# Attention and a mixture of experts on one core: near scores ahead of the last transpose, softmax in halves, first weights loaded in the loop, rows stored at the end

## The chip, the cores and the metric

One core of one Trainium2 chip runs the whole kernel. The time is that of the device, in microseconds (us), from start to end of the program. Short names: PE is TensorE, PEld its weight loads, DVE VectorE, ACT ScalarE, POOL GpSimd, SP SyncE, whose queue issues most transfers.

## The reference, cut to what matters

Two stages, in float32. The attention has 4 batches, 8 heads, 576 positions and heads of 64; it adds a pooled attention (q, k and v averaged over 4 positions, 144 x 144 scores) and a near one (each position sees those less than 4 away). The mixture routes each of 2304 rows to one of 8 experts.

```python
q_d, k_d, v_d = (mean of 4 positions of q, k, v)
out_up = np.repeat(sm_attn(q_d, k_d, v_d), 4, axis=2)
scores = np.where(abs(i - j) < 4, scale * q @ k.T, -1e9)
x = out_up + softmax(scores) @ v            # (4, 576, 512)
logits = x @ w_gate                          # 8 experts, and a local gate
e = argmax(logits) or the previous row's e, by the local gate
out = p[e] * (relu(x @ w1[e]) @ w2[e])       # w1 512 x 1024, w2 1024 x 512
```

## The kernel before, in words

The attention is cut into 16 units, each a batch and a pair of heads. `body(u)` stands once on each engine: unit 0 is written out, units 1 to 14 run in a loop of two bodies, unit 15 is written out. The engines run side by side and meet only at semaphores; on each engine the order is that of the code.

On PE a body is: pool scores of u (L1153); transposes 0 and 1 of unit u+1 (q of the two heads, L1143); near values of u-1 (L1232); transpose 2 (k); the near mask laid into PSUM (L1169); transpose 3; near scores of u on top of the mask (L1179); pool transposes (L1193); `repeat` of u-1 (L1244), which spreads the pooled output over 4 positions; pool values (L1217); near transposes (L1203). Transpose g writes the PSUM bank of its head, so transpose 2 waits for the copies of transpose 0 and transpose 3 for those of transpose 1.

ACT copies the transposes out (L656 for q, four copies a unit; L658 for k, two), takes the exponentials (`exp_pool` L664, `exp_near` L671) and copies their transposes (`pool_out` L678, `near_out` L684). DVE takes maximum and difference of the pool scores (L822, L825) and of the near ones (L833, L836), scales outputs (L857, L846) and adds both outputs into `xs` (`x_out`, L867). POOL adds four neighbours for pooled q and k (`pool_qk`, L489 and L491, once for q and once for k) and v (`pool_v`, L501, L505), and splits the pooled output (`split_opool`).

Every product whose left rows are `float32` and must be exact is made of two parts, hi and lo. The weights of expert 0 are loaded into `w_ring` (`load_w1(0)` L367, `load_w2(0)` L373), and their split runs in 8 pieces of 1024 columns: `first_hi` on ACT (L726), then `first_lo` on POOL (L591). Their place is that of the attention's buffers, so piece 0 waits until q and k of all units are transposed. Between attention and experts stand the logits: 32 steps, each a transpose (`x_chunk`, L1307), a copy on ACT (L732), a difference on DVE (L921) and a product (L1317); every fourth a product back (L1325). Then a chain of small DVE operations finds each row's slot, POOL gathers rows from `x_rows` (L601), and PE runs the experts (L1405). `x_rows` is written by 48 stores of SP (L409).

`keep_warm` (L1126) is a number of products that nobody reads; WARM, WARM_FIRST and WARM_TILES say how many.

Of the kernel before, what the change touches and what calls it, by code (L numbers as in the profile page):

```python
# [34 lines left out]
def build(nc, q, k, v, w_gate, w_local, w1, w2, out):  # L35
# [3 lines left out]
    POOL = 4  # L39
# [56 lines left out]
    WARM, WARM_FIRST, WARM_TILES = 12, 6, 16  # L96
# [3 lines left out]
    with ctx:  # L100
# [159 lines left out]
        s_qk_in = [sem("s_qk_in0"), sem("s_qk_in1")]  # L260
# [62 lines left out]
        def _(sp):  # L323
            def load_qk(u, par):

                wait(sp, s_tr, 4 * (u - 1))
                for h in range(2):
# [3 lines left out]
                                 ).then_inc(s_qk_in[par], 16)  # L331
                for h in range(2):
                    sp.dma_start(k_in[:, par, :, h, :],
                                 ku[one(u), h, :, :].rearrange("o (t p) d -> p (o t) d", p=QT)
                                 ).then_inc(s_qk_in[par], 16)
# [51 lines left out]
            with sp.Fori(2, UNITS // 2) as kk:  # L387
# [6 lines left out]

            sp.dma_start(gates_w[:, :, 0:E], w_gate.rearrange("(c p) e -> p c e", p=128)).then_inc(s_wg, 16)
# [37 lines left out]
        def _(pool):  # L433
# [45 lines left out]
            def pool_qk(u, par):  # L479

                for a in range(2):

                    wait(pool, s_tr_out, COPIES * u + copied[2 * a + 1])
                    if isinstance(u, int) and u == 0:
                        pool.wait_ge(s_tr_odd, a + 2)
# [35 lines left out]
            pool_qk(0, 0)  # L521
# [62 lines left out]
            split_opool(UNITS - 1)  # L584
            constants()

            for i in range(FPIECES):
# [3 lines left out]
                nc.gpsimd.tensor_tensor(lo, lo.bitcast(F32), hi.bitcast(F32), ALU.subtract).then_inc(s_first_lo, 1)  # L591

# [53 lines left out]
        def _(act):  # L646
# [20 lines left out]
            def exp_near(u):  # L667

                wait(act, s_cenn, u + 1)
                wait(act, s_ptn, 2 * u)  # L670
                nc.scalar.activation(p_near[:, :, :, 0:WIN].rearrange("p t h w -> p h t w"), cen_near[:],  # L671
                                     ACT.Exp, scale=SCALE).then_inc(s_expn, 1)

            def pool_out(u):
                wait(act, s_opool, u)
                for h in range(2):
                    wait(act, s_ptp, 2 * u + h + 1)
                    nc.scalar.copy(pt_pool[:, h, :], bank[TBANK[h]][0:PC + 1, 0:GW]).then_inc(s_ptp_out, 1)  # L678
# [7 lines left out]

            def body(u, par, t=True):
# [28 lines left out]
            def first_hi(i):  # L716

                at = i * FCOL
                act.wait_ge(s_w1_in if at < W1C else s_w2_in, 16)
                if i == 0:  # L720
# [772 lines left out]
```

## Time and profile before

| | us |
|---|---|
| runs: median (lowest to highest) of 3 | 500.35 (500.07 to 501.8) |
| the profiled execution: its own time, its span | 502.7, 501.0 |
| start to the end of body 0 | 19.5 |
| bodies 1 to 14 (the loop) | 107.1 |
| body 15 until the last `x_out` | 18.3 |
| logits | 24.4 |
| routing until the first expert product | 29.8 |
| experts | 301.8 |

The stages are cut where PE or DVE begins the next one's first instruction. PE is busy 92% of the span, DVE 51%, ACT 43%, POOL 38%. A time in a row is counted from the start of the span; "L" is a line of the kernel before.

### The profile page before, as it was taken

The numbers are of one execution on the slowest core, as the hardware profiler recorded it, in microseconds if no ns is written. First come the engines' busy times: TensorE is split into PE (matmuls) and PEld (weight loads), VectorE is DVE, ScalarE is ACT, GpSimd is POOL, SyncE is SP. The second block draws the span as 40 slices with busy tenths as digits, with TensorE's granted clock in tenths as the row PEclk, the third lists the DMA queues.
The fourth block names the chain that finished last, engine by engine and source line by source line (L and its number), as shares of the span: only waits on it lengthen the run. The fifth ranks groups of instructions, "written<-read, shape, count | busy, mean of one in ns | idle before, by whom it ended". The sixth has DMA issues, their size and how long they took to land.

```text
span 501.0 us, 13091 instructions
## 1 busy us (share of the span) xinstructions
PE 462.3 (92%) x4156; PEld 371.0 (74%) x4163; DVE 257.0 (51%) x383; ACT 217.3 (43%) x377; POOL 192.7 (38%) x252
## 2 busy tenths in 40 slices
PE   7999999999889558999999999999999999999981
PEld 3787787788667325788888888888888888888860
DVE  3577777677556686353453452345346473522220
ACT  2666767767347220254244252525427282512220
POOL 7777677676459202113204213221321514042200
PEclk9999999999889867999999999999999999999997
DMA  8866665664966732215326421642646564121100
GB/s 179 171 151 161 174 159 149 172 155 92 353 175 149 253 122 43 22 44 211 139 90 230 146 82 48 211 153 78 211 156 231 170 245 156 69 73 35 36 26 6
DMA packets 85936, 69.22 MB, mean 138 GB/s; under 512 B 47886, under 2 KB 70926, under 8 KB 85904
## 3 DMA queue, kind: packets, MB, share of 16 engines
q1 hardware_dynamic: 81408, 57.78, 39.3%
q0 software_dynamic: 4496, 11.03, 7.1%
q8 instruction: 18, 0.29, 0.2%
q14 instruction: 14, 0.11, 0.1%
HBM read 59.34 MB, written 10.76 MB: 140 GB/s over the span
## 4 chain that ended last, share of the span: by engine, by line
PE 77%; DVE 9%; ACT 7%; issue 5%; POOL 1%; ACTq 0%; POOLq 0%; DVEq 0%
PE psum L1405 51%; PE psum L1423 4%; ACT early L656 4%; PE psum L1143 3%; PE psum L1126 3%; PE psum L1203 2%; DVE early L836 2%; DVE top_near L833 2%; PE psum L1179 2%; ACT early L671 2%; PE psum L1153 2%; PE psum L1383 2%; PE psum L1307 2%; PE psum L1317 1%; PE psum L1325 1%
## 5 line engine op out<-in xcount | busy, mean ns | idle before, releaser
L1405 PE MATMUL psum<-w_ring,xg_t 128*128 x552 | 133.9, 398 | 2.3 <-DVE xg_t L1065 1.6
L1405 PE MATMUL psum<-w_ring,h_t 128*128 x552 | 134.3, 398 | 1.9 <-issue 1.9
L1405 PEld LDWEIGHTS psum<-w_ring,xg_t 128*128 128x128 f32 x552 | 102.2, 188 | 25.0 <-issue 2.7
L1405 PEld LDWEIGHTS psum<-w_ring,h_t 128*128 128x128 f32 x552 | 102.0, 188 | 25.0 <-issue 2.4
L607 POOL DMA_INDIRECT out<-tile_bufs,to_row x23 | 23.5, 1024 | 197.3 <-DVE tile_bufs L1080 197.3
L1053 DVE TENSOR_TENSOR w_ring<-w_ring (+1 forms) x28 | 62.9, 2287 | 25.8 <-ACT w_ring L746 25.8
L767 ACT ACTIVATE tile_bufs<-psum 128x512 f32<-128x512 f32 x46 | 25.0, 596 | 86.9 <-PE psum L1405 86.8
L1065 DVE TENSOR_TENSOR xg_t<-psum,xg_t 128x512 fp32r<-128x512 f32 x24 | 16.5, 690 | 84.1 <-ACT xg_t L760 84.1
L746 ACT CAST w_ring<-w_ring (+1 forms) x28 | 52.1, 1910 | 17.4 <-DMA w_ring<-moe_w 17.4
L774 ACT CAST h_t<-psum 128x512 fp32r<-128x512 f32 x46 | 24.8, 591 | 76.3 <-PE psum L1423 76.2
L1080 DVE TENSOR_SCALAR tile_bufs<-psum,slot_w 128x512 f32<-128x512 f32 x23 | 17.2, 749 | 58.2 <-PE psum L1405 58.2
L601 POOL DMA_INDIRECT tile_bufs<-x_rows,from_row x24 | 26.0, 1083 | 36.3 <-DVEq L1020 27.1
L615 POOL DMA_INDIRECT slot_w<-w_rows,from_row x23 | 26.2, 1137 | 17.5 <-DMA w_rows<-weight 10.7
L489 POOL TENSOR_TENSOR early<-early 128x288 f32<-128x288 f32 x32 | 21.3, 665 | 26.3 <-ACT early L656 22.8
L656 ACT COPY early<-psum 64x288 f32<-64x288 f32 x60 | 25.0, 417 | 13.9 <-PE psum L1143 12.8
L1071 DVE TENSOR_TENSOR h_t<-psum,h_t 128x512 fp32r<-128x512 f32 x46 | 29.5, 683 | 2.1 <-ACT h_t L774 1.8
L1143 PE MATMUL psum<-ident,early 96*128 96x96 f32 x192 | 27.1, 263 | 1.9 <-ACT early L707 0.2
L1143 PEld LDWEIGHTS psum<-ident,early 96*128 96x128 f32 x192 | 18.4, 143 | 12.0 <-ACT early L656 6.0
L1423 PE MATMUL psum<-ident,tile_bufs 128*128 128x128 f32 x184 | 23.9, 273 | 0.3 <-ACT tile_bufs L767 0.3
L1423 PEld LDWEIGHTS psum<-ident,tile_bufs 128*128 128x128 f32 x184 | 21.4, 141 | 3.7 <-ACT tile_bufs L767 0.5
L1126 PE MATMUL psum<-warm 128*128 128x512 bf16 x60 | 21.5, 516 | 2.4 <-POOL warm L441 1.4
L760 ACT CAST xg_t<-psum 128x512 fp32r<-128x512 f32 x24 | 14.2, 593 | 19.2 <-PE psum L1383 19.2
(179 smaller groups left out, 613.4 us busy)
## 6 DMA issues: line engine op xcount, KB each, us to landing
w_ring<-moe_w SPq DMA_DIRECT2D x16, 2048.0 KB, 9.1
early<-q SPq DMA_DIRECT2D x32, 144.0 KB, 2.5
early<-k SPq DMA_DIRECT2D x32, 144.0 KB, 3.1
early<-v SPq DMA_DIRECT2D x16, 288.0 KB
x_rows<-early SPq DMA_DIRECT2D x48, 96.0 KB, 2.5
early<-v SPq DMA_DIRECT2D x32, 120.0 KB
early<-v SPq DMA_DIRECT2D x64, 13.5 KB
early<-v SPq DMA_DIRECT2D x32, 15.0 KB
```

The source lines that it names most:

```text
L601: pool.indirect_dma_start(xg[:, t % 2, :], None, x_rows[:, :], bass.IndirectOffsetOnAxis(from_row[:, t:t + 1], 0), bounds_check=NTOK - 1, ...
L615: pool.indirect_dma_start(slot_w[:, t:t + 1], None, w_rows[:, :], bass.IndirectOffsetOnAxis(from_row[:, t:t + 1], 0), bounds_check=NTOK - ...
L656: nc.scalar.copy(q_of(par, g, e), q_transposed(g, e)).then_inc(s_tr_out, 1)
L746: nc.scalar.copy(w_ring[:, bass.ds(at + i * n, n)], w_ring[:, bass.ds(at + (WCOLS + i * n), n)].bitcast(F32)).then_inc(s_hi, 1)
L767: nc.scalar.activation(h_act[:, n * 512:(n + 1) * 512], bank[1 + n][:, :], ACT.Relu).then_inc(s_relu, 1)
L774: nc.scalar.copy(h_t[:, 0, n * 512:(n + 1) * 512], bank[3 + n][:, :]).then_inc(s_ht_hi, 1)
L1053: nc.vector.tensor_tensor(part, part.bitcast(F32), w_ring[:, bass.ds(at + i * n, n)].bitcast(F32), ALU.subtract).then_inc(s_lo, 1)
L1071: nc.vector.tensor_tensor(h_t[:, 1, n * 512:(n + 1) * 512], bank[3 + n][:, :], h_t[:, 0, n * 512:(n + 1) * 512].bitcast(F32), ALU.subtract ...
L1126: mm(bank[b][:, :], warm[:, 0:128], warm[:, :], start=True, stop=True)
L1143: last = nc.tensor.transpose(bank[TBANK[h]][:, j * QT:(j + 1) * QT], rows, ident[0:QT, 0:QT])
L1405: ins = mm(bank[b][:, :], rows, w_ring[:, bass.ds(at + (off + c * width + n * 512), 512)], start=(c == 0 and k == 0), stop=(c == chunks - ...
L1423: last = nc.tensor.transpose(bank[3 + n][:, c * 128:(c + 1) * 128], h_act[:, (4 * n + c) * 128:(4 * n + c + 1) * 128], ident[:])
```

## The change

- Near scores follow the mask at once; transpose 3 comes behind them.
- Maximum, difference and exponential of the near scores run in two halves of three tiles; on ACT `pool_out` and `exp_near` alternate by halves, on PE the near transposes and the pool values wait by halves, and `repeat` is cut around the pool transposes.
- q and k have semaphores of their own, so the first q transposes don't wait for k.
- DVE makes the pooled q and k of unit 0, in place of POOL.
- Eight in place of twelve opening warm-up products, four in place of six in each of two places of body 0 (the second cut into two and two).
- `load_w1(0)` and `load_w2(0)` are issued between turns of the load loop, behind the loads of units 7 and 11. `first_hi` 0 to 2 run in body 15, 3 to 5 early in the logits, 6 and 7 behind the logits' exponential; `first_lo` 0 and 1 run ahead of the last `split_opool`.
- All 48 stores wait for the last `x_out`; before, those of a batch waited for that batch.

```diff
-    WARM, WARM_FIRST, WARM_TILES = 12, 6, 16
+    WARM, WARM_FIRST, WARM_TILES = 8, 4, 16
...
+            with sp.Fori(2, 4) as kk:
+                two_units(kk)
+            load_w1(0)
+            with sp.Fori(4, 6) as kk:
+                two_units(kk)
+            load_w2(0)
+            with sp.Fori(6, UNITS // 2) as kk:
+                two_units(kk)
...
-            load_w1(0)
-            load_w2(0)
...
+            sp.wait_ge(s_x, UNITS)
             for b in range(NB):
-                wait(sp, s_x, HP * (b + 1))
...
-            pool_qk(0, 0)
             pool_v(0, 0, 0)
...
+            first_lo(0)
+            first_lo(1)
+            split_opool(UNITS - 1)
+            constants()
+            for i in range(2, FPIECES):
+                first_lo(i)
...
+            def exp_near(u, j):
+                tiles = slice(j * HALF, (j + 1) * HALF)
+                wait(act, s_cenn, 2 * u + j + 1)
                 wait(act, s_ptn, 2 * u)
...
+                else:
+                    first_hi(0)
                 exp_pool(u)
+                if not t:
+                    first_hi(1)
...
-                pool_out(u)
-                exp_near(u)
+                for j in range(2):
+                    pool_out(u, j)
+                    exp_near(u, j)
+                if not t:
+                    first_hi(2)
                 near_out(u)
...
+                if k == 1:
+                    first_hi(3)
+                    first_hi(4)
+                elif k == 8:
+                    first_hi(5)
             act.wait_ge(s_cent, 1)
...
+            first_hi(6)
+            first_hi(7)
...
+                for j in range(2):
+                    tiles = slice(j * HALF, (j + 1) * HALF)
+                    nc.vector.reduce_max(top_near[:, :, tiles], s4[:, :, tiles], X).then_inc(s_topn, 1)
+                    wait(dve, s_topn, 2 * u + j + 1)
+                    nc.vector.tensor_tensor(cen_near[:, :, tiles], s4[:, :, tiles],
...
+            for a in range(2):
+                dve.wait_ge(s_tr_out, copied[2 * a + 1])
+                dve.wait_ge(s_tr_odd, a + 2)
+                t4 = qk_t[:, 0, a, :].rearrange("p (s r) -> p s r", r=POOL)
+                nc.vector.tensor_tensor(qk_part[:, a, :, :], t4[:, :, 0:2], t4[:, :, 2:4], ALU.add).then_inc(s_part, 1)
...
                 near_masked(u, par)
+                near_scores(u, par)
                 if t:
                     transposes(3, u + 1, 1 - par, nxt)
-                near_scores(u, par)
-                pool_transposes(u, t)
-                if x:
-                    repeat(u - 1)
-                else:
-                    keep_warm(WARM_FIRST, 7)
+                for j in range(2):
+                    if x:
+                        repeat(u - 1, j, HALF if j else 1)
+                    else:
+                        keep_warm(WARM_FIRST // 2, 7)
+                    pool_transposes(u, j, t)
                 pool_values(u, par)
                 near_transposes(u)
```

PE's order in a body of the loop, before, from the mask (L1169) to the pool transposes and `repeat` (L1244); `L32` rows are waits' registers:

```order
L1169 MATMUL psum<-mask,ident_b 112x324 x2
L32 REGISTER_ALU
L1143 MATMUL psum<-ident,early 128x96 x3
L1179 MATMUL psum<-early 48x54 x24
L32 REGISTER_ALU
L1193 MATMUL psum<-ident,early 72x72 x2
L1193 MATMUL psum<-ident,early 73x72 x2
L32 REGISTER_ALU
L1193 MATMUL psum<-ident,early 72x72 x2
L1193 MATMUL psum<-ident,early 73x72 x2
L1244 MATMUL psum<-o_pool_r,rep_r 112x256 x6
```

The same place now; mask L1209, near scores L1219, transpose L1183, `repeat` L1284, pool transposes L1232:

```order
L1209 MATMUL psum<-mask,ident_b 112x324 x2
L1219 MATMUL psum<-early 48x54 x24
L32 REGISTER_ALU
L1183 MATMUL psum<-ident,early 128x96 x3
L1284 MATMUL psum<-o_pool_r,rep_r 112x256 x2
L32 REGISTER_ALU
L1232 MATMUL psum<-ident,early 72x72 x2
L1232 MATMUL psum<-ident,early 73x72 x2
L1284 MATMUL psum<-o_pool_r,rep_r 112x256 x4
L32 REGISTER_ALU
L1232 MATMUL psum<-ident,early 72x72 x2
L1232 MATMUL psum<-ident,early 73x72 x2
```

The 24 near scores moved ahead of a transpose of 3, and one third and two thirds of `repeat` stand before the first and the second half of the pool transposes.

ACT's order now in body 15 and the first logit steps; L712 is `first_hi`, L691 `pool_out`, L685 `exp_near`, L697 `near_out`, L754 the logits' copy:

```order
L712 CAST w_ring<-w_ring 128x1024
L691 COPY pt_pool<-psum 73x288
L685 ACTIVATE early<-early 112x2x3x54
L691 COPY pt_pool<-psum 73x288
L685 ACTIVATE early<-early 112x2x3x54
L712 CAST w_ring<-w_ring 128x1024
L697 COPY pt_near<-psum 128x336 x2
L754 CAST x_t<-psum 128x288 x2
L712 CAST w_ring<-w_ring 128x1024 x2
L754 CAST x_t<-psum 128x288 x7
L712 CAST w_ring<-w_ring 128x1024
L754 CAST x_t<-psum 128x288 x23
```

Before, the pieces (L726) stood one by one between the logits' copies (L732), up to the last of them:

```order
L726 CAST w_ring<-w_ring 128x1024
L732 CAST x_t<-psum 128x288 x3
L726 CAST w_ring<-w_ring 128x1024
L732 CAST x_t<-psum 128x288 x5
L737 ACTIVATE expo<-e_buf 112x192
```

Three pieces moved up into body 15, three stand early in the logits, two fall behind L737.

## Rows read from the trace of the kernel before

**Rows 1.** Busy time by stage: length, engines (PE first), granted clock, DMA share, GB/s.

```profile
0.00:19.52 19.52, 15.66 (x139) 9.34 (x142) 7.60 (x19) 7.98 (x18) 13.88 (x36) 1.00 0.87 181
19.52:126.61 107.09, 102.62 (x2158) 85.64 (x2160) 79.48 (x126) 73.36 (x167) 77.79 (x115) 1.00 0.63 152
126.61:144.91 18.30, 15.78 (x234) 12.34 (x237) 10.06 (x18) 6.23 (x15) 6.37 (x25) 0.81 0.92 310
144.91:169.35 24.44, 22.04 (x178) 17.59 (x177) 14.44 (x36) 16.69 (x34) 18.95 (x8) 1.00 0.57 139
```

**Rows 2.** Chain that ended last, one body of the loop: start, us, what.

```profile
91.85 0.76 PE psum L1179 x48
...
92.64 0.84 DVE top_near L833
...
94.37 0.76 ACT early L671
```

**Rows 3.** Timeline of PE, the same body.

```profile
90.82 0.44 PE L1169 MATMUL psum<-mask,ident_b 112*112 112x324 bf16 x2
91.38 0.47 PE L1143 MATMUL psum<-ident,early 96*128 96x96 f32 x3
...
93.85 1.19 PE L1217 MATMUL psum<-v_pool,pt_pool 72*72 72x65 f32 x16
95.25 0.79 PE L1203 MATMUL psum<-ident,early 112*128 112x112 f32 x6 [0.20 <-ACT early L671]
95.97 0.47 PE L1153 MATMUL psum<-early 64*72 64x144 f32 x4
```

**Rows 4.** Timeline of ACT and DVE, the same body.

```profile
91.35 0.69 ACT L664 ACTIVATE early<-early 72x576 f32<-72x576 f32 x1
...
90.88 0.96 DVE L857 TENSOR_TENSOR o_near<-psum,r_near 112x768 f32<-112x768 f32 x1
```

**Rows 5.** Timeline, start of the kernel.

```profile
1.40 5.30 PE L1126 MATMUL psum<-warm 128*128 128x512 bf16 x12 [1.40 <-POOL warm L441]
...
8.79 0.46 DVE L899 COPY early<-psum 128x288 f32<-128x288 f32 x1 [0.62 <-PE psum L1143]
...
10.88 0.71 PE L1153 MATMUL psum<-early 64*72 64x144 f32 x8 [1.26 <-POOL early L491]
...
19.52 0.71 PE L1153 MATMUL psum<-early 64*72 64x144 f32 x8 [0.84 <-POOLq L535]
```

**Rows 6.** Chain that ended last, body 15 and the logits.

```profile
132.68 1.28 issue
133.96 1.11 PE psum L1217 x8
...
139.25 1.47 PE psum L1232 x48
...
155.28 0.28 ACT w_ring L726
```

**Rows 7.** Transfers that SP issued, in order of time.

```profile
110.00 0.83 SPq L329 DMA_DIRECT2D early<-q  x2
...
125.15 3.49 SPq L409 DMA_DIRECT2D x_rows<-early  x1
...
154.98 9.74 SPq L409 DMA_DIRECT2D x_rows<-early  x15
166.75 0.37 SPq L367 DMA_DIRECT2D w_ring<-moe_w  x1
```

**Rows 8.** Timeline, logits to the first gather.

```profile
144.55 1.05 ACT L726 CAST w_ring<-w_ring 128x1024 fp32r<-128x1024 f32 x1
...
174.69 1.90 ACT L746 CAST w_ring<-w_ring 128x2048 fp32r<-128x2048 f32 x1 [3.78 <-DMA w_ring<-moe_w]
...
193.29 1.26 POOL L601 DMA_INDIRECT tile_bufs<-x_rows,from_row  x1 [27.09 <-DVEq L1020]
...
197.62 0.58 ACT L760 CAST xg_t<-psum 128x512 fp32r<-128x512 f32 x1 [19.23 <-PE psum L1383]
```

More of the change, by code:

```diff
@@ L386, in _, with two_units @@
             load_v_raw(3, 1)
-            with sp.Fori(2, UNITS // 2) as kk:
+            def two_units(kk):
                 load_v_win(2 * kk - 2, 0)
@@ L583, in _, with first_lo @@
             pool.sem_inc(s_gates, 1)
-            split_opool(UNITS - 1)
-            constants()
-            for i in range(FPIECES):
+            def first_lo(i):
                 pool.wait_ge(s_first_hi, i + 1)
@@ L685, in near_out, with first_hi @@
                                    bank[TBANK[j]][:, 0:TW]).then_inc(s_ptn_out, 1)
+            def first_hi(i):
+                at = i * FCOL
+                act.wait_ge(s_w1_in if at < W1C else s_w2_in, 16)
+                if i == 0:
+                    act.wait_ge(s_tr, 4 * UNITS)
+                elif i == 3:
+                    act.wait_ge(s_vpool, UNITS)
+                    act.wait_ge(s_pooled, 2 * UNITS)
+                elif i == 6:
+                    act.wait_ge(s_onear, UNITS)
+                nc.scalar.copy(w_ring[:, at:at + FCOL],
+                               w_ring[:, WCOLS + at:WCOLS + at + FCOL].bitcast(F32)).then_inc(s_first_hi, 1)
             def body(u, par, t=True):
@@ L733, in _ @@
                                rows_of(bank[XBANK[k]])).then_inc(s_xt_hi, 1)
-                if k % 3 == 2 and 4 <= k and k // 3 - 1 < FPIECES:
-                    first_hi(k // 3 - 1)
+                if k == 1:
[3 more added lines that the diff above has]
+                    first_hi(5)
             act.wait_ge(s_cent, 1)
@@ L1128, in transposes @@
             def transposes(g, u, par, half):
-                wait(pe, s_qk_in[par], 64 * (half + 1))
                 if g < 2:
+                    wait(pe, s_q_in[par], 32 * (half + 1))
                     wait(pe, s_ptn_out, 2 * (u - 2) + g + 1)
                 else:
+                    wait(pe, s_k_in[par], 32 * (half + 1))
                     wait(pe, s_tr_out, COPIES * u + copied[g - 2])
@@ L1146, in pool_scores @@
             def pool_scores(u, par):
-                wait(pe, s_cenn, u)
+                wait(pe, s_cenn, 2 * u)
                 wait(pe, s_pooled, 2 * u + 2)
@@ L1208, in pool_values @@
             def pool_values(u, par):
-                wait(pe, s_ptp_out, 2 * u + 2)
                 wait(pe, s_vpool, u + 1)
                 wait(pe, s_onear_out, u)
-                for qc in range(2):
-                    for h in range(2):
+                for h in range(2):
+                    wait(pe, s_ptp_out, 2 * u + 1 + h)
+                    for qc in range(2):
                         c0 = (qc * 2 + h) * VW
@@ L1235, in near_values, with repeat @@
                 last.then_inc(s_onear, 1)
-            def repeat(u):
-                wait(pe, s_osplit, 2 * u + 2)
-                wait(pe, s_x, u)
-                for i in range(HALF):
+            def repeat(u, first=0, end=HALF):
+                if first == 0:
+                    wait(pe, s_osplit, 2 * u + 2)
+                    wait(pe, s_x, u)
+                for i in range(first, end):
                     for part in range(2):
@@ L1245, in repeat @@
                                   o_pool_r[:, part, :], start=(part == 0), stop=(part == 1))
-                last.then_inc(s_rep, 1)
+                if end == HALF:
+                    last.then_inc(s_rep, 1)
             def body(u, par, half, t=True, x=True):
@@ L1340, in _ @@
             pe.wait_ge(s_gates, 1)
-            pe.wait_ge(s_cenn, UNITS)
+            pe.wait_ge(s_cenn, 2 * UNITS)
             logit_step(0, 1)
```

70 lines of the change are left out of this document (27 added, 43 removed).

## The prediction

> **What bounds the kernel now.** I cut the profile by stages first, since the edits sit in four of them [rows 1]. The start takes 19.52 us, the loop 107.09 for 14 bodies (7.65 each), body 15 until the last sum into xs 18.30, the logits 24.44. The reader is to see PE busy 102.62 of 107.09 in the loop. So a body has little idle PE time to give back, and PE's own work is the floor of whatever is gained there.
>
> Second, the chain of waits inside a body. It leaves PE at the end of the near scores (91.85 + 0.76 = 92.61), runs over DVE twice (maximum and difference, 0.84 each), over ACT (0.76), and comes back to PE for the near transposes [rows 2]. PE does other things meanwhile, so third its timeline [rows 3]: where does it really stand still? At two places. The mask starts at 90.82 and the transpose behind it, which waits for ACT's copies of the q transposes, only at 91.38. And the pool values, 1.19 from 93.85, end at 95.04, but the near transposes start at 95.25, released by ACT.
>
> Fourth, body 15, which takes 18.30 where a body of the loop takes 7.65. The reader is to see a hole of 1.28 put down to "issue", in the middle of 16 like products with no wait between them, and behind it products at half speed: the near values take 1.47 [rows 6], and the granted clock of the stage is 0.81 on average [rows 1]. In this stage DMA is at 0.92 of its time and moves 310 GB/s, against 152 in the loop: the two first weight loads, 4 MB, are under way.
>
> **The start.** Twelve warm-up products take 5.30 from 1.40, 0.44 each [rows 5]; eight end 1.7 earlier, near 4.9, and the first transposes no longer wait for k. Their duration at the low clock doubles for the first six, which eats a part, so I put DVE's last copy of k (ends 9.25 [rows 5]) at 7.8. The pooled sums come behind it on DVE. Its price is read from the 288-element copy (0.46 [rows 5]) and the 648-element maximum (0.84 [rows 2]): 1.06 ns an element and 0.15 fixed. Two sums of 288 and two of 144 elements are then 1.5 to 1.6, and pool scores 0 start near 9.5 in place of 10.88: 1.4 gained. Body 1 does not begin by PE's own work: it waits for POOL (L535, at 19.52 [rows 5]), which makes its constants behind the k sums of unit 1, and these now hang on a transpose that comes behind the near scores, some 0.25 later in the body. **1.1 us gained**; bounds 2.0 gained (POOL freed earlier) and 1.0 lost (the clock comes later).
>
> **The loop.** With near scores straight behind the mask, DVE can begin when they end: mask at 90.82 plus about 0.34, near scores 0.76, so 91.92. DVE is busy with `o_near` until 90.88 + 0.96 = 91.84 [rows 4], just in time. Halves of 324 elements cost 0.50 each by the slope above, so the four end at 92.4, 92.9, 93.5 and 94.0; that is 0.33 more DVE work, in a body where it is busy 79.48 / 14 = 5.7 of 7.65. ACT: 576 elements take 0.69 [rows 4] and 648 0.76 [rows 2], so half of them about 0.48. With the `pool_out` halves between, the two exponentials end near 93.8 and 94.65. PE meanwhile: transpose 3 (0.47 less an overlap of 0.07), pool transposes, `repeat` and pool values, which before took from 92.61 to 95.04, 2.43. They end at 91.92 + 0.40 + 2.43 = 94.75. The first near transposes need the first exponential (93.8), the second, begun near 95.1, the second (94.65). So neither of the two stops is left, with 0.4 to spare at the tighter one.
>
> What PE gains is its idle time and no more. First stop: 0.56 from start to start in place of 0.34, 0.2. Second: 1.40 from start to start in place of 1.19 less the 0.07 by which modelled ends overlap the next start (95.25 + 0.79 against 95.97 [rows 3]), 0.28. I take 0.45 of the 0.5, since waits are now taken by halves: 7.20 a body, **6.3 us gained** over 14. Bounds: only the first stop goes (0.2, so 2.8) and 0.6 a body (8.4). Transpose 3 itself comes later by near scores, but its copy on ACT stands behind the pool exponential, which ends at 91.35 + 0.69 = 92.04 [rows 4], and one k copy, so 92.4 as before: no cost while that cover stands, at most 0.4 of POOL's slack if not.
>
> **Body 15.** The weights are now loaded behind units 7 and 11, eight and four bodies ahead of where their neighbours in the queue stood, so DMA is nearly idle here. I take the 1.28 hole for something that full DMA queues cause, instructions that come late among them, and the low clock for its consequence; the trace shows them only together. Laid out with the durations of the loop, PE ends the near transposes 7.3 after the body's start. `first_hi` 0 and 1 (1.05 each [rows 8]) fall in ACT's idle time before and behind the pool exponential. `first_hi` 2 does not: it holds `near_out` until 8.5. Then one logit transpose (0.45), four warm-ups (0.9, at half their opening 0.44 each) and near values (0.83, a little over half of the 1.47) end at 10.7. From there to the last `x_out` it took 144.91 - 140.72 = 4.2 before, and nothing there changes. 14.9 against 18.3: **3.4 us gained**. Bounds: 0.5 and 4.5. `first_lo` 0 and 1 hold the last `split_opool` by some 2 us, hidden by near values, as `repeat` 15 comes two logit steps later.
>
> **The logits.** ACT carries 8 pieces of 1.05 among 32 copies, and twice the chain runs over such a piece [rows 6, 8]. The first costs about its 1.05; at the second a group of four steps takes some 0.7 longer. Now two pieces stand before near values end, one at the ninth copy, and two behind the exponential where ACT waits anyway. **1.7 us gained**; bounds 1.0 and 2.5.
>
> **The late stores.** The last `x_out` would end at 144.9 - 1.1 - 6.3 - 3.4 = 134.1. An undisturbed store costs 9.74 / 15 = 0.65 of SP [rows 7]; 48 end at 165.3. Before, w1 of expert 1 was issued 2.0 behind the last store, and ACT began to split it at 174.69, 7.9 later [rows 7, 8]. So ACT splits from 175.2 to 179.0. It is needed for the first gathered rows at 197.62 - 12.5 = 185.1, and the gather itself at 180.8 needs stores landed by then; they have been since 167. Nothing lost, with 6 us to spare; without that cover each 0.1 a store costs 4.8.
>
> **Sum.** 1.1 + 6.3 + 3.4 + 1.7 = 12.5. The profiled execution took 502.7, its span 501.0, so it becomes 490.2. It stands 2.35 above the median of the runs, 500.35; the forecast for the median is 487.9.
>
> **Rivals.**
> - *The hole in body 15 stays.* For it: the cut is inside straight-line code just behind a loop, which the change keeps. Against: the like code of the logits has no such hole, at 139 GB/s. Then 1.28 and the half-speed products behind it return, together the 3.4, and the gain is 9.1: 491.3. The Trainium skill (Runtime: NRT & Kernel Launch, Instruction fetch mechanics) says that the fetch of the next block of straight-line code is mostly hidden, which would speak for another cause and so for this rival; the row shows the hole and not what it waited for.
> - *Halves cost what they give.* More instructions and waits on DVE and ACT keep one PE stop: 0.2 a body, gain 9.0: 491.4. Against: DVE has over a microsecond idle in a body.
> - *The weights push the units' loads.* Each is 2.1 MB, 6.8 us at the 310 GB/s of the stage that had them [rows 1]. q of unit 15 was issued at 110.00 [rows 7] and is used in body 14, which starts at 126.61 - 7.65 = 118.96, 0.64 in. Less 0.8 to issue and 2.5 to land (the page's median for q) 6.3 are spare, 5.4 at the new pace. SP itself was held 3.49 by the two loads [rows 7]. If both add up, 3.5 + 6.8 - 5.4 = 4.9 a load: 497.7. The Trainium skill (DMA: Bandwidth & Descriptors, Queues, rings and completion order) says that an engine takes descriptors in ring order; by it whatever follows a weight waits for all of it. Against the full sum: q is issued some 5 us behind the weight, so most of it has passed.
> - *The clock comes late.* Eight warm-ups may not carry it through body 0; it then runs at 1.2 GHz and costs some 5: 493. The rows show only that twelve did.
> - *The late stores decide,* the one on the other side. Stores, landing, load and split of expert 1's w1 then stand ahead of ACT's first gathered rows. It turns the sign at (197.6 - 3.8 - 7.9 - 2.0 - 134.1) / 48 = 1.04 a store. For it: the first store took 3.49 [rows 7]. Against: that was behind 4 MB, and fifteen free ones took 0.65 each. At 1.15 a store, 505 for the profiled execution: 503.
>
> **Chances.** Forecast 0.66, the hole 0.12, halves 0.08, pushed loads 0.07, late clock 0.04, late stores 0.03. The first three rivals and the unknown costs of the loop (-2.1 to +3.5) set the range: 483.5 to 495.5. What a measurement of this kernel tells from no change is about 0.5%, 2.5 us. Pushed loads at nearly their full price end within it, and so does a late clock with a second rival; the late stores end above. Faster 0.91, same 0.06, slower 0.03.
>
> **What would show it.** Body to body 7.2 in the loop; no PE stop before the near transposes; four DVE rows of about 0.50 with 324 elements; transposes starting near 4.9 and pool scores near 9.5; no hole in body 15 and a granted clock near 1.0 there; DMA full for 5 to 6 us twice in the loop with PE unmoved; stores from about 134 to 165 and 9 us or more between their landing and the first gather. The prediction is wrong if PE waits for loads in the loop, if PE's order costs more than the sum of its products, or if the expert stage starts by ACT's split and not by the gather.

## The result, and the profile after

The changed kernel takes 507.39 us (median of 20 runs, 501.23 to 517.76) against 500.28 for the kernel before (20 runs, 499.13 to 503.05). Its range is four times as wide. The ratio is 1.0085, interval 1.0059 to 1.0110; it leaves out the executions that lie over 1.5% above the fastest of their kernel (7 of the 20 here; the median of the other 13 is 504.37), which is why it is smaller than that of the medians. So the change makes the kernel slower, by 0.9%. Where two versions are compared below, the ratios decide, and a difference of medians stands beside them only to tell the size.

The profiled execution took 504.37, its span 502.6, against 502.7 and 501.0 before. It lies 3 us below the median of all 20, so the trace shows a mild case. The mean granted clock of all 20 executions goes with their time: 0.960 in the one of 501.23, 0.922 in the one of 517.76.

The same stages as in [rows 1], kernel after (length; busy time of PE, PEld, DVE, ACT, POOL; granted clock; DMA share; GB/s):

```profile
0.00:18.45 18.45, 13.13 (x132) 8.04 (x134) 9.18 (x25) 8.11 (x19) 11.71 (x32) 1.00 0.89 177
18.45:128.66 110.21, 105.11 (x2158) 88.86 (x2158) 82.84 (x154) 76.78 (x181) 77.26 (x114) 0.94 0.85 186
128.66:143.46 14.80, 13.11 (x235) 10.39 (x237) 10.41 (x21) 10.63 (x21) 12.80 (x29) 1.00 0.01 2
143.46:166.47 23.01, 21.84 (x178) 17.58 (x177) 14.49 (x35) 11.18 (x27) 8.22 (x4) 1.00 0.54 133
```

| stage | before | after | difference |
|---|---|---|---|
| start, until body 1 | 19.52 | 18.45 | -1.07 |
| bodies 1 to 14 | 107.09 | 110.21 | +3.12 |
| body 15 until the last sum into xs | 18.30 | 14.80 | -3.50 |
| logits | 24.44 | 23.01 | -1.43 |
| routing, until the first product of expert 0 | 29.82 | 34.36 | +4.54 |
| experts | 301.83 | 301.77 | -0.06 |
| span | 501.0 | 502.6 | +1.6 |

Three stages went as forecast. Two did not: the loop, which should have given 6.3, and the routing, which the prediction did not touch. The reader is to see the loop's granted clock, 0.94 where it was 1.00.

**An undisturbed body.** From body to body the 14 took 9.98, 7.40, 7.17, 7.12, 7.19, 7.13, 8.66, 7.10, 7.18, 7.11, 12.74, 7.11, 7.19 and 7.10. Ten lie between 7.10 and 7.19. PE in one of these, the same place as [rows 3] (start, us, engine, line, operation, output<-inputs, shape, count):

```profile
45.47 0.44 PE L1209 MATMUL psum<-mask,ident_b 112*112 112x324 bf16 x2
45.84 0.79 PE L1219 MATMUL psum<-early 64*48 64x54 f32 x48
...
48.23 1.38 PE L1256 MATMUL psum<-v_pool,pt_pool 72*72 72x65 f32 x16
49.45 0.74 PE L1242 MATMUL psum<-ident,early 112*128 112x112 f32 x6
```

and DVE's four halves in the same body:

```profile
46.99 0.50 DVE L863 TENSOR_REDUCE top_near<-psum 112x6 f32<-112x324 f32 x1 [0.51 <-PE psum L1219]
47.52 0.50 DVE L865 TENSOR_TENSOR early<-psum,top_near 112x324 f32<-112x324 f32 x1
47.94 0.48 DVE L863 TENSOR_REDUCE top_near<-psum 112x6 f32<-112x324 f32 x1
48.45 0.49 DVE L865 TENSOR_TENSOR early<-psum,top_near 112x324 f32<-112x324 f32 x1
```

No bracket of a wait stands on the PE rows: both stops of before are gone, and a half costs the 0.50 that was forecast.

**The three long bodies.** PE's timeline of after; the bracket gives the idle time ahead of the row and what ended it:

```profile
18.45 1.24 PE L1193 MATMUL psum<-early 64*72 64x144 f32 x8 [2.27 <-POOLq L543]
...
20.77 1.55 PE L1271 MATMUL psum<-early,pt_near 55*48 55x65 f32 x48
...
66.32 0.86 PE L1183 MATMUL psum<-ident,early 96*128 96x96 f32 x6 [1.16 <-DMA early<-q]
67.11 0.90 PE L1271 MATMUL psum<-early,pt_near 55*48 55x65 f32 x48
...
98.65 1.22 PE L1183 MATMUL psum<-ident,early 96*128 96x96 f32 x6 [3.45 <-DMA early<-q]
99.80 1.55 PE L1271 MATMUL psum<-early,pt_near 55*48 55x65 f32 x48
```

Two of the three wait for q. The near values (L1271) take 0.90 in a free body. Behind the first and the third stop they take 1.55, as in other stretches at a granted clock of 0.50, and behind the second 0.90. So the stop of 1.16 costs its body only 8.66 - 7.15 = 1.5, with a wait of 0.24 for k behind it, and the stop of 3.45 costs 12.74 - 7.15 = 5.6: the wait, and the products at 1.2 GHz behind it. Why q is late stands in SP's timeline of after, behind the first weight load (L367):

```profile
52.53 0.41 SPq L367 DMA_DIRECT2D w_ring<-moe_w  x1
...
54.26 0.94 SPq L356 DMA_DIRECT2D early<-v  x2
55.38 2.22 SPq L350 DMA_DIRECT2D early<-v  x2
57.79 1.07 SPq L356 DMA_DIRECT2D early<-v  x2
59.14 2.74 SPq L329 DMA_DIRECT2D early<-q  x2
```

and in the windows of after around both loads (columns as above):

```profile
50.00:55.00 5.00, 5.00 (x130) 4.02 (x128) 3.89 (x7) 4.06 (x10) 3.35 (x6) 1.00 1.03 201
55.00:60.00 5.00, 5.00 (x96) 4.23 (x94) 4.26 (x10) 3.66 (x10) 4.09 (x6) 1.00 1.01 354
60.00:65.00 5.00, 5.00 (x97) 4.31 (x95) 4.05 (x8) 4.06 (x10) 4.11 (x7) 1.00 1.23 220
65.00:70.00 5.00, 3.60 (x115) 2.78 (x112) 2.77 (x5) 2.81 (x7) 2.37 (x5) 1.00 0.94 160
...
97.00:103.00 6.00, 4.35 (x83) 3.52 (x87) 1.19 (x2) 2.73 (x6) 1.09 (x2) 0.50 0.91 175
```

The weight itself costs SP only 0.41. But from about 55 to 61 the DMA engines move 284 to 397 GB/s where they moved 183 in the body before (44.3 to 51.5), and issuing a pair of q loads takes 2.74 where it took 0.83 [rows 7]. This q is that of unit 8: it is issued 6.6 behind the weight and ends the stop at 66.32, 4.4 behind the end of its issue, where the median of all q loads is 2.9. The DMA share by itself tells less. It stands at 0.94 or more from 50 to 70, but it was 0.90 in the body before the load, and in e7 (below) the same unit loads show 0.92 for 25 us, from 41 to 66, with no pair of issues over 1 us and no stop of PE. The last row has the granted clock around the second stop for q, 0.50.

**The routing.** POOL and DVE of after, just behind the logits:

```profile
169.05 4.64 POOL L597 TENSOR_TENSOR w_ring<-w_ring 128x1024 fp32r<-128x1024 f32 x2 [17.36 <-ACT w_ring L712]
169.06 2.37 DVE L992 TENSOR_TENSOR keep<-keep,later 112x24 f32<-112x24 f32 x1
171.46 2.25 DVE L993 TENSOR_SCALAR keep<-keep,valid 112x24 f32<-112x24 f32 x1
173.75 0.18 DVE L994 TENSOR_TENSOR fresh<-fresh,keep 112x24 f32<-112x24 f32 x1
```

The same two operations, in the kernel before:

```profile
171.94 0.18 DVE L953 TENSOR_TENSOR keep<-keep,later 112x24 f32<-112x24 f32 x1
172.16 0.24 DVE L954 TENSOR_SCALAR keep<-keep,valid 112x24 f32<-112x24 f32 x1
```

POOL's two operations are the residuals (`first_lo`) of pieces 6 and 7, which the change puts behind the logits' exponential. Each DVE operation begins beside one of them (2.34 the first, and 4.64 both) and lasts until it ends: 4.62 for what took 0.42. These 4.2 are nearly the whole of the stage's +4.54.

**The late stores.** SP, ACT and POOL of after:

```profile
143.48 33.25 SPq L420 DMA_DIRECT2D x_rows<-early  x48
178.82 0.40 SPq L367 DMA_DIRECT2D w_ring<-moe_w  x1
...
186.71 3.70 ACT L772 CAST w_ring<-w_ring 128x2048 fp32r<-128x2048 f32 x2 [16.80 <-DMA w_ring<-moe_w]
...
194.84 1.26 POOL L614 DMA_INDIRECT tile_bufs<-x_rows,from_row  x1 [21.15 <-DVEq L1059]
```

48 stores take 33.25 / 48 = 0.69 each. ACT's split ends at 190.4, and the first gather starts at 194.84 behind DVE, so neither stores nor split decide in this trace.

### The profile page after: what moved, and what is told of

The parts are those of the page before. It is cut to its first block, busy times and chain, and to the rows that moved or that the text cites. A ratio compares the mean times of both kernels' runs of the same rounds, so it can differ in the third digit from the quotient of the medians.

```text
span 502.6 us, 13207 instructions
## 1 busy us (share of the span) xinstructions
PE 459.0 (91%) x4148; PEld 371.1 (74%) x4155; DVE 267.3 (53%) x419; ACT 221.5 (44%) x393; POOL 189.8 (38%) x248
## 4 chain that ended last, share of the span: by engine, by line
PE 73%; SPq 11%; DVE 6%; issue 4%; DMA 3%; POOL 1%; ACT 1%; POOLq 0%; DVEq 0%
PE psum L1447 51%; PE psum L1465 4%; SPq L356 3%; SPq L350 3%; PE psum L1425 2%; PE psum L1183 2%; SPq L329 2%; PE psum L1349 2%; SPq L333 2%; PE psum L1271 2%; PE psum L1359 1%; PE psum L1256 1%; DMA early<-v 1%; PE psum L1367 1%; PE psum L1219 1%
## 5 line engine op out<-in xcount | busy, mean ns | idle before, releaser
L1183 PE MATMUL psum<-ident,early 96*128 96x96 f32 x192 | 28.5, 273 | 5.3 <-DMA early<-q 4.6
L498 POOL TENSOR_TENSOR early<-early 128x288 f32<-128x288 f32 x30 | 20.0, 665 | 28.1 <-ACT early L669 20.3
L1183 PEld LDWEIGHTS psum<-ident,early 96*128 96x128 f32 x192 | 19.2, 149 | 12.7 <-issue 8.7
L597 POOL TENSOR_TENSOR w_ring<-w_ring 128x1024 fp32r<-128x1024 f32 x8 | 18.7, 2364 | 17.7 <-ACT w_ring L712 17.4
L1256 PE MATMUL psum<-v_pool,pt_pool 72*72 72x65 f32 (+1 forms) x256 | 22.1, 231 | 0.2 <-ACT pt_pool L691 0.2
```

The costliest lines, as they stand in the source:

```text
L1183: last = nc.tensor.transpose(bank[TBANK[h]][:, j * QT:(j + 1) * QT], rows, ident[0:QT, 0:QT])
L1256: last = mm(bank[4][0:PC, c0:c0 + VW], pt_pool[0:PC + c, h, at:at + PC], v_pool[0:PC + c, par, h, c, :], start=(c == 0), stop=(c == 1))
```

## The experiments

The theory had three parts: the two weight loads in the loop cost most, by late q loads and the clock that falls behind them (the late loads); the last two residuals hold DVE, 4.2 us (the held DVE); PE's stop before body 1 lets the clock fall, 2.8 us (the early stop). Against it stood that the new order of the loop costs the time itself, and, for the late loads, that only the order within SP's queue is at fault, or only the size of a transfer. The kernel before ran beside each of them, with medians of 500.19 (the first four runs), 500.21 (the next two), 500.57 (the next four) and 500.75 (the last two).

| run | median | range, runs | ratio to before, interval |
|---|---|---|---|
| e1_weights_back | 492.73 | 491.01 to 499.97, 6 | 0.9848, 0.9802 to 0.9894 |
| e2_split_early | 503.20 | 497.43 to 508.26, 12 | 1.0012, 0.9979 to 1.0046 |
| e3_reps_first | 504.41 | 500.93 to 511.40, 12 | 1.0057, 1.0028 to 1.0086 |
| e4_pieces | 500.20 | 499.01 to 505.58, 12 | 1.0015, 0.9986 to 1.0044 |
| e5_before_loads | 505.80 | 504.39 to 506.37, 6 | 1.0108, 1.0088 to 1.0127 |
| e6_all_three | 499.16 | 492.51 to 501.52, 6 | 0.9892, 0.9854 to 0.9931 |
| e7_repairs | 490.48 | 489.97 to 491.44, 5 | 0.9804, 0.9782 to 0.9827 |
| e8_stores_staged | 490.79 | 488.92 to 491.20, 5 | 0.9801, 0.9777 to 0.9826 |
| e9_act_queue | 509.71 | 502.84 to 513.72, 8 | 1.0066, 1.0035 to 1.0097 |
| e11_warm_back | 495.02 | 493.76 to 498.13, 6 | 0.9893, 0.9864 to 0.9923 |
| e12_loop_alone | 494.15 | 493.96 to 495.65, 6 | 0.9879, 0.9857 to 0.9902 |

**e1: the weight loads and their splits where they were before, the rest of the change kept.**

```diff
-            with sp.Fori(2, 4) as kk:
-                two_units(kk)
-            load_w1(0)
-            with sp.Fori(4, 6) as kk:
-                two_units(kk)
-            load_w2(0)
-            with sp.Fori(6, UNITS // 2) as kk:
+            with sp.Fori(2, UNITS // 2) as kk:
                 two_units(kk)
...
             load_v_win(UNITS - 1, 1)
+            load_w1(0)
+            load_w2(0)
...
+                if k % 3 == 2 and 4 <= k and k // 3 - 1 < FPIECES:
+                    first_hi(k // 3 - 1)
```

> The changed kernel with the first weight loads and all eight first splits back where the kernel before has them (loads behind the load loop, pieces among the logits); late stores and everything else of the change stay. Theory A (the weight loads in the loop hold up q and k of later units, and two of the late split pieces on POOL stretch two tiny DVE operations to 2.4 and 2.3 us): no PE wait for q in the loop, bodies 2 to 14 all 7.1 to 7.2 us, the two tiny DVE operations back at 0.2 us; body 15 again near 18 us with its hole; profiled execution near 497.5 us, and the times of its runs within 1% of each other. Rival B (the loop reordered by halves is itself what stalls, by PE waits that wander): single bodies of 8 to 13 us stay, and the time stays above 502. Rival C (nothing but SP's own pace holds the loop): bodies between 7.2 and 7.6 with SP never waiting.

Measured: 492.73, 14.7 below the changed kernel by the medians and 2.4%, some 12 us, by the ratios. No wait for q or k is left in the loop, and 12 of its 14 bodies take 7.11 to 7.19. The two DVE operations take 0.18 and 0.24 again. The run takes away the late loads and the held DVE together and does not price them apart. SP's timeline of e1 up to the q of the same unit 8:

```profile
59.40 0.76 SPq L350 DMA_DIRECT2D early<-v  x2
60.34 0.80 SPq L356 DMA_DIRECT2D early<-v  x2
61.41 0.83 SPq L329 DMA_DIRECT2D early<-q  x2
```

This q is issued 7.9 ahead of body 7, which uses it, and in after only 5.3 ahead. The new order of the loop is that of the changed kernel, and it pays. The early stop shows too: PE still stops 2.51 before body 1, and in the traced execution (499.97, above the median) the clock stays down for two bodies, 11.83 and 9.92. A body 15 near 18 did not come: it takes 14.97.

**e2: pieces 6 and 7 split at the 13th and 17th copy of the logits.**

```diff
-                elif k == 8:
-                    first_hi(5)
+                elif k in (8, 12, 16):
+                    first_hi({8: 5, 12: 6, 16: 7}[k])
...
-            first_hi(6)
-            first_hi(7)
```

> The changed kernel with first_hi 6 and 7 moved from behind the logits' exponential to the 13th and 17th logit copy, so that POOL has split the last piece before the routing begins. Theory A: the DVE operations of lines 992 and 993 (0.2 us each in the kernel before, 2.38 and 2.27 in the changed one) last as long because POOL works at two pieces then; they are back at 0.2, routing takes 29.8 us in place of 34.4, and the logits at most 0.7 more: 4 us off the changed kernel's profiled 504.4. Rival: they wait for something else that runs at that time (ACT's copies of the same pieces, or code that comes late): the two stay at 2.3 each and nothing is gained.

Measured: 503.20, 4.2 below the changed kernel by the medians and 3.7 by the ratios, whose intervals lie apart. The routing takes 29.69 in place of 34.36, the two operations 0.18 and 0.24, and the logits stay at 23.05, where after had 23.01. So the held DVE is shown, and the split could have gone early at no price. The loop has its q waits as before, of 1.49 and 3.17.

**e3: POOL makes the constants of `repeat` ahead of the first pooled v.**

```diff
-            pool_v(0, 0, 0)
-            pool_qk(1, 1)
-
             grid = rep[:].rearrange("p t (s r) -> p t s r", s=2)[:, :, :, 0:QS]
...
             pool.sem_inc(s_reps, 1)
+
+            pool_v(0, 0, 0)
+            pool_qk(1, 1)
```

> The changed kernel with POOL's repeat constants made while POOL waits for v of unit 0, ahead of its first pool_v. Theory A: PE stood still 2.27 us before body 1 because POOL made them behind the k sums of unit 1, and that idle time is what dropped the clock to 1.2 GHz for body 1 (10.05 us in place of 7.15): body 1 starts near 16.2 in place of 18.45 and takes 7.2 to 7.6 at full clock; 4.5 to 5 us off, unless the loads of the loop then take some of it back. Rival: the clock falls anyhow, for want of the warm-up products taken out (4 and 6 fewer): body 1 starts near 16.2 and still takes 10.

Measured: 504.41; the ratio, 1.0057, is not clearly apart from that of the changed kernel. Body 1 starts at 16.37 without a stop and takes 7.20, so the early stop has its cause in POOL's order. But the late loads take this back in the trace: body 7 starts 4.9 earlier than in after, the q that it needs is issued only 3.0 earlier, at 56.14. PE's timeline of e3:

```profile
64.15 1.22 PE L1183 MATMUL psum<-ident,early 96*128 96x96 f32 x6 [3.90 <-DMA early<-q]
...
67.31 0.74 PE L1209 MATMUL psum<-mask,ident_b 112*112 112x324 bf16 x2
```

The wait was 1.16 in after; here it is 3.90, the mask behind it takes 0.74 in place of 0.44, and the body 15.76.

**e4: each weight load in four pieces of 512 KB, one behind the loads of each of units 6 to 13.**

```diff
-            load_w1(0)
...
+                if i is not None:
+                    piece(i)
```

> The changed kernel with each first weight load cut into four of 512 KB, one issued behind the loads of each of units 6 to 13. Theory A (a 2 MB load in the queue holds back what is issued behind it, and PE then waits for q): no q wait over 0.5 us in the loop and no fall of the clock there, 7 us off, and runs closer together than 501 to 518. Rival (SP's queue has no room for 4 MB more in the loop however it is cut: 6.5 us of issuing a unit in a body of 7.2): SP falls behind piece by piece, and a wait of some us returns in bodies 10 to 14; less than 3 us off.

Measured: 500.20. More waits (0.53, 0.48, 1.38 and 1.56), none as long as 3.45, and bodies 10 to 13 take 8.19, 8.62, 11.99 and 9.55. Against the changed kernel this is 7.2 less by the medians but 3.5 by the ratios, about half of the 7 that were expected if size alone were at fault. So a smaller transfer helps, but the backlog is spread and not removed.

**e5: the kernel before, with only its two weight loads moved into the load loop.**

```diff
+            with sp.Fori(2, 4) as kk:
+                two_units(kk)
+            load_w1(0)
+            with sp.Fori(4, 6) as kk:
+                two_units(kk)
+            load_w2(0)
```

> The kernel before with one edit: the two first weight loads issued in the load loop, at the places of the change. Its bodies take 7.65 us, so q of a unit has about 0.9 us more to spare than in the changed kernel, and the splits stay among the logits. Theory A on the hole in body 15 (full DMA queues cause it): the hole of 1.28 us and the low clock behind it are gone, body 15 takes 14.5 to 15.5 in place of 18.3; on the loop: the second load still makes PE wait once, for 1 to 4 us. Together 497 to 502. Rival: the hole belongs to straight-line code behind the loop and stays, body 15 stays at 18.3, and the time is 500 to 504.

Measured: 505.80, 5.6 above the kernel before. This is the cost of the loads alone, in a loop whose bodies of 7.65 give q and k half a microsecond more each, and more than the 497 to 502 expected. Two waits for k stand in its trace, of 0.48 and 2.46, in bodies of 8.20 and 12.23. Body 15 has no hole there and takes 14.69, near the 14.86 of the second trace of before (e10). PE's and SP's timelines of e5:

```profile
92.64 1.88 SPq L329 DMA_DIRECT2D early<-q  x2
...
100.62 1.22 PE L1150 MATMUL psum<-ident,early 96*128 96x96 f32 x6 [2.46 <-DMA early<-k]
```

**e6: the edits of e2, e3 and e4 together.**

> The changed kernel with all three repairs: late pieces earlier, repeat constants first, weight loads in pieces of 512 KB. If theory A holds and nothing new comes up: body 1 near 16.2 at full clock, 14 bodies of 7.2, body 15 14.8, logits 23.3, routing 29.8, experts 301.8, sum 486.7 and 1.8 around it: 488.5 profiled. Rival: with a shorter body SP, whose issues take 6.5 us a unit and more with weights, is the bound; bodies from 10 on near 7.5 or with a wait, 491 to 496.

Measured: 499.16, with a wide range; neither expectation came. The trace is of one of its long executions, 500.78. One q wait of 1.44 is left in it, and behind it three bodies of 12.36, 12.32 and 9.81. With the held DVE and the early stop repaired and the loads in pieces, what follows this single short stop still costs 5.21 + 5.17 + 2.66 = 13 us against three bodies of 7.15. The lowest execution, 492.51, lies 8.3 below and can't have lost all of it.

**e7: the edits of e1 and e3 together.**

> Weights and their first splits back at the places of the kernel before, and the repeat constants made ahead of pool_v; the rest as changed. Theory A: no wait for q, no PE stop before body 1, so no fall of the clock: body 1 near 16.4, bodies of 7.1 to 7.2, body 15 from about 116.5, logits from there as in the run with the weights back (39.4 us later): span near 485.5, profiled 487.5, median 486 to 488.5, runs within 3 us of each other. Rival: the clock falls at some other place once the first stop is gone, and the median stays at 491 to 493.

Measured: 490.48, with a range of 1.5 us; no version is faster, and the expected 486 to 488.5 was missed by 2. PE at the start of body 1, and the windows of body 15, in e7:

```profile
16.29 0.71 PE L1175 MATMUL psum<-early 64*72 64x144 f32 x8
```

```profile
116.63:123.00 6.37, 5.91 (x136) 4.69 (x138) 4.97 (x10) 2.62 (x7) 2.80 (x8) 1.00 0.97 376
123.00:131.31 8.31, 7.36 (x102) 5.82 (x102) 5.53 (x12) 3.69 (x10) 4.19 (x18) 1.00 0.55 207
```

All bodies take 7.10 to 7.40. In the first 6.4 of body 15 the DMA engines are as full as in [rows 1], 0.97 for 0.92, and yet there is no hole over 0.2 and the clock is 1.00: it takes 14.68. Against the second trace of before (e10, below), body 1 starts 4.2 earlier, bodies 1 to 14 take 6.7 less, body 15 0.2 less, and the logits and the routing 1.8 more: 9.3, where the spans differ by 498.4 - 489.0 = 9.4. Of the 1.8, 1.6 stand in the logits (25.98): there the granted clock fell to 0.50 for some us (135 to 137), with no stop over 0.71 ahead of it and no trace that says why.

**e8: e7, with the stores waiting batch by batch as before.**

```diff
-            sp.wait_ge(s_x, UNITS)
             for b in range(NB):
+                wait(sp, s_x, HP * (b + 1))
```

> The kernel of e7_repairs with the stores of rows again waiting batch by batch, as before, so that they are issued right behind the weight loads during body 15. Theory A: the late stores cost and gain nothing, since routing waits for neither way: within 1 us of e7_repairs. Rival B: stores among the end of the attention are what made the hole of 1.28 us and the low clock in body 15 of the kernel before: then that hole is back here, and the time is 2 to 4 us above e7_repairs.

Measured: 490.79 against 490.48. The late stores neither cost nor give, and the early ones bring back no hole of 1.28 (0.24 in the trace) and no long body 15 (14.95).

**e9: the changed kernel, with the weight loads issued by ACT's own queue, behind bodies 6 and 10.**

```diff
+            with act.Fori(0, 3) as kk:
+                body(2 * kk + 1, 1)
+                body(2 * kk + 2, 0)
+            act.dma_start(w_ring[:, WCOLS:WCOLS + W1C].bitcast(F32).rearrange("p (c f) -> p c f", c=KD),
+                          w1.rearrange("e (c p) f -> e p c f", p=128)[0, :, :, :]).then_inc(s_w1_in, 16)
```

> The changed kernel with the two first weight loads issued by ACT, behind bodies 6 and 10, on a queue of their own, in place of SP's. If the harm comes from standing in the same queue (q behind 2 MB, SP held), the waits for q in the loop are gone or below 0.5 us, and 5 to 7 us come off the changed kernel. If it comes from the DMA engines being busy (0.6 to 0.7 of their time go to the units' small packets, so 5.7 us more work takes some 17 to drain, whatever the queue), q still lands late and PE waits 1 us or more at least once, with the clock falling behind it: 500 to 506.

Measured: 509.71, ratio 1.0066 against 1.0085 by SP, with intervals that overlap: no better by ACT's queue. The trace is of one of its longest executions, 513.13. The windows of e9 behind the first load, issued at 67.84:

```profile
70.00:75.00 5.00, 5.00 (x96) 4.36 (x97) 4.40 (x9) 4.06 (x11) 3.63 (x6) 1.00 1.02 382
75.00:80.00 5.00, 3.26 (x115) 2.58 (x111) 2.65 (x4) 3.17 (x8) 2.89 (x5) 1.00 1.19 200
80.00:90.00 10.00, 10.00 (x118) 8.85 (x108) 5.21 (x11) 4.85 (x12) 4.61 (x7) 0.53 1.00 186
```

SP issues no weight here, and its pairs of loads still take up to 2.86 in place of 0.8, PE still waits (1.74 for k), and three bodies of 10.99, 12.33 and 9.81 follow. Behind ACT's second load, at 108.14, SP's pairs take up to 2.45 and PE doesn't stop. So the waits don't need the weight in the queue of q and k; the time of the DMA engines is what is left. The Trainium skill says as much (DMA: Bandwidth & Descriptors, Issuing engines are not separate DMA queues): transfers of all issuing engines run on the same DMA engines. The trace agrees, by the shares of 1.02 and 1.19 above. The ring rule that the prediction weighed isn't needed for it.

**e11: e1 with the warm-up products of before (twelve, and six twice).**

```diff
-    WARM, WARM_FIRST, WARM_TILES = 8, 4, 16
+    WARM, WARM_FIRST, WARM_TILES = 12, 6, 16
```

> The kernel of e1_weights_back with the warm-up products as before (12, 4, 6 and 3+3). Theory A (the idle stop before body 1, and not the number of warm-ups, lets the clock fall): the start costs 1 to 2 us more and body 1 still falls to 1.2 GHz in some executions: 493 to 495. Rival: the missing warm-ups are what lets it fall, and it never does now: 490 to 492, with body 1 at 7.2 to 7.7 in the profile.

Measured: 495.02, 2.3 more than e1 by the medians, with intervals of the ratios that overlap. Body 1 starts at 20.84, 1.9 later than in e1, and still takes 8.52, behind a stop of 1.11. So fewer warm-ups start the loop earlier, and they are not why the clock falls.

**e12: the kernel before, with only the new order of the loop: near scores behind the mask, halves, semaphores of their own for q and k.**

> The kernel before with one part of the change: near scores ahead of transpose 3, softmax in halves, repeat and waits by halves (and q and k on semaphores of their own). Warm-ups, first sums, constants, weights, splits and stores as before. Theory A: 14 bodies of 7.1 to 7.2 in place of 7.65, 6.5 to 7 us, all of it kept, as nothing is loaded in the loop: median 493 to 494.5 if the stop before body 1 stays short. Rival: the start is where the reordered body is fragile: pool constants come later by the later k sums, PE stops for more than 1 us before body 1 and the clock falls for it, 496 to 499 with a wide spread.

Its loop is that of the changed kernel, its load order, splits, start and stores those of the kernel before. Measured: 494.15 against 500.75, so 6.6 gained. The bodies take 7.10 to 7.21, body 1 too, though PE stops 1.11 before it, as in e11, where body 1 took 8.52.

**e10: the kernel before once more, for a second trace of it (500.25).**

> The kernel before once more, for a second trace of it. If the hole of 1.28 us in body 15 and the low clock behind it belong to each execution, both are there again within 0.3 us. If they wander (the runs with the weights behind the loop showed 0 to 0.9 us there), its length differs, and so does the granted clock of body 15.

Its chain through body 15, and that stage's window:

```profile
133.02 0.58 PE psum L1217 x8
133.59 0.39 issue
133.98 0.67 PE psum L1217 x8
```

```profile
127.46:142.32 14.86, 13.50 (x238) 10.31 (x237) 10.08 (x18) 6.13 (x15) 6.50 (x26) 1.00 0.99 348
```

The hole is 0.39 and not 1.28, the clock is 1.00, and the stage takes 14.86 where the first trace had 18.30. The weights are in flight in both, with DMA at 0.99 here.

## Why the prediction was wrong

The forecast was 487.9, its range ended at 495.5, and the median is 507.39. The step that failed is that of the pushed loads, put at nothing; beside it the sum left out the residuals on POOL, and booked 3.4 in body 15 that the kernel before does not lose in each execution. By its own steps:

**The start, 1.1 gained: 1.07 measured,** but a part of this match is luck: in the second trace of before (e10) body 1 starts at 20.46, 2.0 later than in after. The pooled sums of 288 and 144 elements took 0.45 and 0.31 on DVE, pool scores 0 started at 8.76 (forecast 9.5). What it missed is the stop: body 1 "waits for POOL" stood there as a reason why the gain is small, and not as an idle time of 2.27 behind which the clock falls. What followed it cost 9.98 - 7.15 = 2.8 in the trace. Nor was it the warm-ups, of which the rival of the late clock spoke (e11). e7 shows what the stage holds: body 1 at 16.29 and at full clock.

**The loop, 7.20 a body: right in mechanism and size,** 7.15 where nothing disturbs it, and 6.6 gained by e12 where 6.3 was forecast. The rival of costly halves is out.

**Pushed loads, the step that failed.** The prediction had this rival, with a full price of 4.9 a load, and put it aside by "q is issued some 5 us behind the weight, so most of it has passed". That reckons with an idle DMA: 2.1 MB at 310 GB/s, 6.8 us. But the loop's own small transfers already took 0.63 of the DMA engines' time [rows 1]. If what is free is 0.37, then 6.8 us of work fills 6.8 / 0.37 = 18 us, two and a half bodies. This is an estimate made afterwards, and a rough one, as the share of the same unit loads was 0.83 in the loop of e7. The rows show what came of it: q of unit 8 ends PE's wait 4.4 behind its issue, where 2.5 were reckoned, and SP, whose issues fill some 6.5 us of an undisturbed body of 7.15, falls behind as they stretch from 0.83 to 2.74. Which of the two weighs more no run separates. The second half of the price was missing too: some stops are followed by products at 1.2 GHz (that of 1.16 is not), so that one of 3.45 costs 5.6, and one of 1.44 was followed by bodies 13 us longer in all (e6). The runs show each part: e5 adds 5.6 by the loads alone, e1 takes the waits away, and e9 has them without the weight in SP's queue. The prediction's sign of being wrong, "if PE waits for loads in the loop", is the one that came.

**Body 15, 3.4 gained: the length was right and the gain was not one.** The stage takes 14.8, forecast 14.9. But the kernel before takes 14.9 too in the one other trace of it (e10, an execution of 500.25, at the median): the 18.30 belonged to the execution that was traced. That one stood 2.35 above the median, and at least part of this was the very hole that I took out of it as a gain. Two traces don't say how often it comes. Nor do full DMA queues make it: e7 has them at 0.97 with no hole. A hole was seen only with the weights in flight there (1.28 and 0.39 in the two traces of before, 0.97 in e12, 0.86 in e11, 0.27 in e1, 0.24 in e8, none over 0.2 in e7), and none over 0.2 in the kernels that load them in the loop, e5 among them; what sets its length stays open.

**The logits, 1.7 gained: 1.4 measured,** and none of it with the pieces put back (24.43 in e1). But the term left out what the two pieces behind the exponential start: their residuals on POOL, beside DVE's chain through the routing. That is 4.2 us lost by the two operations, and 4.7 of the stage are back in e2. The price could have been expected. The Trainium skill (SBUF — State Buffer, Who interferes with whom) says that VectorE and GpSimd share a pair of ports, that a VectorE instruction with two inputs in SBUF contends with a GpSimd one that reads SBUF, and that `tensor_scalar` can contend too, where it runs in a mode that uses both ports; the one that comes second is blocked. By that rule the first operation of `keep` waits for POOL's, and the second may; the rows agree for both, since each ends within 0.1 us of one of POOL's.

**The late stores, 0: right,** by e8 against e7, and 0.69 a store against 0.65.

**The sum.** Trace against trace: -1.07 + 3.12 - 3.50 - 1.43 + 4.54 - 0.06 = +1.6. Against the second trace of before (e10): -2.0 for the start, +3.2 for the loop, -0.1, -1.4, +4.6 and -0.1, together +4.2, which is what the ratio says (0.85% of 500). The loop's +3.12 is 7.0 gained by the new order and 2.8 + 1.5 + 5.6 lost in three bodies, and some 0.2 in body 2. The median of all 20 lies 7.1 above that of before. The rest of this, 3 us, stands in executions longer than the traced one, with a lower mean clock (0.922 in the slowest). In which bodies they lose it, no trace shows.

## What to carry to other kernels

Before a bulk load goes into a loop because the bytes are few, read the DMA share of the loop and how full the issuing queue is: the load shares the DMA engines with the small ones, and those behind it are late until it has drained. Count with each PE stop the products at the lower clock that may follow it, in one trace nine times the stop and in others nothing. Keep GpSimd's long operations away from short VectorE operations that a chain runs over, and take a second trace before a hole of one execution is booked as a gain.

## What the runs showed of the hardware that was not expected

- A stop of 1.44 us was followed by some 27 us at half clock (e6: three bodies of 34.49 in place of 21.5; e9 much the same behind 1.74), while stops of 0.53 (e4) and 0.48 (e5) cost about themselves. The granted clock of such a stretch is 0.50 (80 to 104 in e9: 0.53 and 0.50). Which stops end so stays open, and their length alone does not decide: one of 1.16 in after cost 1.5 us in all, one of 1.69 before body 1 in e2 left body 1 at 7.20, and of two of 1.11 before body 1 one left it at 7.21 (e12) and one at 8.52 (e11).
- Issuing slowed down while a large transfer ran, though it stood in another queue: up to 2.86 for a pair of loads in e9, 0.80 else.
- A VectorE operation of 24 elements took 2.37 and one of 2.25, in place of 0.18 and 0.24, beside GpSimd operations of 2.3.
